# Attention tokens on 128 partitions in four and a half columns instead of 96 partitions in six

## The reference

```python
# 1. linear attention, per batch and head
q_s = softmax(q, axis=-1)              # over the 64 numbers of a token
k_s = softmax(k, axis=2)               # over the 576 tokens
attn = q_s @ (k_s.T @ v)               # x: [B, 576, 512]
# 2. token mixing, then channel mixing
h   = relu(x.T @ w_tok1) @ w_tok2      # 576 -> 256 -> 576 over tokens
u   = x + h.T
x1  = u + relu(u @ w_ch1) @ w_ch2      # 512 -> 1536 -> 512
# 3. experts: one of E = 8 per token
logits = x1 @ w_gate; local = sigmoid(x1 @ w_local)
# a token takes argmax(logits) if local < 0.5 (or it is the first), else the expert of the token before
out = softmax(logits)[e] * (relu(x1 @ w1[e]) @ w2[e])
```

## Time and profile before

| | us |
|---|---|
| median of three runs | 767.28 |
| lowest and highest | 767.22, 769.18 |
| profiled execution | 769.06 |
| its span, first to last instruction | 767.3 |

### The profile page before, as it was taken

The page is one execution under the profiler, slowest core; times in us unless marked ns, Lnnn a source line. Parts: engine busy times, 40 slices in busy tenths (PEclk is TensorE's granted clock), DMA queues, the critical chain, the costliest instruction groups (busy, mean ns, idle before and its releaser), DMA issues.

```text
span 767.3 us, 14091 instructions
## 1 busy us (share of the span) xinstructions
PE 748.6 (98%) x4836; PEld 682.4 (89%) x4837; DVE 310.0 (40%) x617; ACT 226.5 (30%) x401; POOL 141.7 (18%) x159
## 2 busy tenths in 40 slices
PE   6999999999999999999999999999999899999997
PEld 6979999999999999999999999977788688888885
DVE  6656251226241226251223643584624363222531
ACT  2753133113123104123103025221624362222531
POOL 6483030002020002020000015102312131212221
PEclk9999999999999999999999999999999999999999
DMA  9950305001405001401001240105723444101010
GB/s 206 372 92 14 81 14 111 1 2 32 94 1 124 1 1 33 93 1 32 1 1 37 81 153 31 52 28 196 266 80 122 159 164 137 49 27 49 18 35 12
DMA packets 67851, 57.62 MB, mean 75 GB/s; under 512 B 51356, under 2 KB 53116, under 8 KB 67808
## 3 DMA queue, kind: packets, MB, share of 16 engines
q1 hardware_dynamic: 64288, 47.57, 21.9%
q0 software_dynamic: 3520, 9.44, 3.7%
HBM read 48.79 MB, written 10.31 MB: 77 GB/s over the span
## 4 chain that ended last, share of the span: by engine, by line
PE 88%; DVE 5%; POOL 2%; ACT 1%; issue 1%; DMA 1%; DVEq 0%; ACTq 0%; SPq 0%; POOLq 0%
PE bank L583 38%; PE bank L729 14%; PE bank L704 14%; PE bank L525 5%; PE bank L554 4%; PE bank L716 2%; POOL qb L1611 2%; PE bank L497 2%; PE bank L548 2%; PE bank L593 1%; PE bank L604 1%; PE bank L652 1%; PE bank L513 1%; PE bank L535 1%; DVE qsum L1087 1%
## 5 line engine op out<-in xcount | busy, mean ns | idle before, releaser
L583 PE MATMUL bank<-u_h,wc_h 128*128 128x288 f32 x384 | 119.9, 312 | 0.0
L583 PE MATMUL bank<-hid_h,wc_h 128*128 128x288 f32 x384 | 116.9, 304 | 0.0
L583 PE MATMUL bank<-hid_l,wc_h 128*128 128x288 f32 x384 | 113.2, 295 | 0.0
L583 PE MATMUL bank<-u_l,wc_h 128*128 128x288 f32 x384 | 113.1, 294 | 0.0
L583 PE MATMUL bank<-hid_h,wc_l 128*128 128x288 f32 x384 | 113.0, 294 | 0.0
L583 PE MATMUL bank<-u_h,wc_l 128*128 128x288 f32 x384 | 113.0, 294 | 0.0
L704 PE MATMUL bank<-wslots,xgT_h 128*128 (+1 forms) x344 | 110.5, 402 | 0.4 <-issue 0.2
L729 PE MATMUL bank<-wslots,hT_h 128*128 (+1 forms) x336 | 105.1, 394 | 5.2 <-DVE hT_l L1504 5.2
L1331 DVE SCALAR_TENSOR_TENSOR hid_l<-bank,hid_h 128x288 fp32r<-128x288 f32 x96 | 43.4, 454 | 128.2 <-ACT hid_h L883 128.0
L729 PEld LDWEIGHTS bank<-wslots,hT_h 128*128 128x128 f32 x336 | 63.0, 189 | 19.9 <-issue 4.4
L883 ACT ACTIVATE hid_h<-bank 128x288 fp32r<-128x288 f32 x96 | 39.0, 408 | 124.7 <-PE bank L583 124.7
(11 more groups left out here) (247 smaller groups left out, 1080.4 us busy)
## 6 DMA issues: line engine op xcount, KB each, us to landing
w1raw<-in_moe_w_dram SPq DMA_DIRECT2D x20, 512.0 KB, 5.0
w2raw<-in_moe_w_dram SPq DMA_DIRECT2D x20, 512.0 KB, 3.7
wc_raw<-in_moe_w_ch_dram SPq DMA_DIRECT2D x8, 768.0 KB, 11.1
x_rows<-x1n SPq DMA_DIRECT2D x24, 192.0 KB, 2.1
kb<-in_k_dram SPq DMA_DIRECT2D x24, 144.0 KB, 3.4
qb<-in_q_dram SPq DMA_DIRECT2D x24, 144.0 KB, 3.3
vb_e<-in_v_dram SPq DMA_DIRECT2D x16, 144.0 KB, 3.9
vb_o<-in_v_dram SPq DMA_DIRECT2D x16, 144.0 KB, 3.7
```

The costliest lines, as they stand in the source:

```text
L583: last = pe.matmul(to, lhsT, rhs, start=(m == 0), stop=(m == len(mms) - 1))
```

## The change

Tokens stand on all 128 partitions. The first 512 tokens of a batch fill four columns (partition p holds tokens 4p to 4p+3), and the last 64 stand on partitions 0 to 63 of a fifth column. `TOP` = 4 is that column's number, `FULL` = 512, `REST` = 64. The parts of the softmaxes are now columns 0 to 1 and 2 to 4. Products over tokens use 128 rows for four columns and 64 for the fifth (`tokens_on`). In `qT` the tokens now stand as two halves of 256 + 32, in order of the token within each: the half with tokens 0 to 255 and 512 to 543, and the one with 256 to 511 and 544 to 575. ACT's copies out of PSUM do this ordering, and the rows of a half come out as two blocks of 128 and one of 32 in plain token order.

The core of the diff, with the rest left out:

```diff
-    PS = 96
-    NI = S // PS
-    HI = NI // 2
+    NI = -(-S // P)
+    TOP = NI - 1
+    FULL = TOP * P
+    REST = S - FULL
+    HB = 3
+    NB = 2 * HB
...
-        IHALF = (slice(0, HI), slice(HI, NI))
+        IHALF = (slice(0, 2), slice(2, NI))
+        BLOCKS = ((0, P), (P, P), (2 * P, REST // 2))
+        def tokens_on(i):
+            return P if i < TOP else REST
...
             def load_raw(dst, src, g, b, landed):
-                sp.dma_start(dst[:, g, :, :, :].rearrange("p h i d -> p h (i d)"),
-                             src[b, g * HG:(g + 1) * HG, :, :].rearrange("h (p i) d -> p h (i d)", p=PS)).then_inc(landed, 16)
+                heads = src[b, g * HG:(g + 1) * HG, :, :]
+                sp.dma_start(dst[:, g, :, 0:TOP, :].rearrange("p h i d -> p h (i d)"),
+                             heads[:, 0:FULL, :].rearrange("h (p i) d -> p h (i d)", p=P)).then_inc(landed, 16)
+                sp.dma_start(dst[0:REST, g, :, TOP, :], heads[:, FULL:S, :].rearrange("h p d -> p h d")).then_inc(landed, 16)
...
             def store_logits(b):
                 sp.wait_ge(lg_done, 2 * b + 3)
-                rows = lg_rows.rearrange("(b p i) r -> b p (i r)", b=B, i=NI)
-                rows = rows[bass.ds(b, 1), :, :].rearrange("a p n -> (a p) n")
-                sp.dma_start(rows, lgs[:, :, :].rearrange("p i r -> p (i r)")).then_inc(lg_stored, 16)
+                for half in range(2):
+                    at = b * S + block_row(half * HB)
+                    sp.dma_start(lg_rows[at:at + 2 * P, :].rearrange("(k p) r -> p k r", k=2), lgs[:, half, 0:2, :]).then_inc(lg_stored, 16)
+                    at, size = b * S + block_row(half * HB + 2), BLOCKS[2][1]
+                    sp.dma_start(lg_rows[at:at + size, :], lgs[0:size, half, 2, :]).then_inc(lg_stored, 16)
...
             def kv(n, g):
...
-                        last = pe.matmul(k_bank(n, g)[:, c * KV:(c + 1) * KV], keys(n)[:, i, c * P:(c + 1) * P], vb[g][:, 2 * c:2 * c + 2, i, :],
+                        last = pe.matmul(k_bank(n, g)[:, c * KV:(c + 1) * KV], keys(n)[0:tokens_on(i), i, c * P:(c + 1) * P], vb[g][0:tokens_on(i), 2 * c:2 * c + 2, i, :],
...
             def qT_out(n, g, tiles):
                 for j in tiles:
                     act.wait_ge(qT_ready, 4 * n + j + 1)
-                    act.activation(qT[:, g, j // 2, HS * (j % 2):HS * (j % 2) + HS], bank[4 + j % 2][:, 0:HS], ACT.Copy).then_inc(qT_done, 1)
+                    halves = qT[:, g, j // 2, :].rearrange("p (h s) -> p h s", h=2)
+                    in_order = halves[:, :, 0:2 * P].rearrange("p h (q i) -> p i h q", i=TOP)[:, 2 * (j % 2):2 * (j % 2) + 2, :, :]
+                    done = act.activation(in_order, bank[4 + j % 2][:, 0:2 * P].rearrange("p (i h q) -> p i h q", i=2, h=2), ACT.Copy)
+                    if j % 2:
+                        done = act.activation(halves[:, :, 2 * P:HS], bank[5][:, 2 * P:2 * P + REST].rearrange("p (h q) -> p h q", h=2), ACT.Copy)
+                    done.then_inc(qT_done, 1)
...
         def _(pool):
...
+            for i, raw in enumerate((qraw, kraw)):
+                pool.memset(raw[REST:P, :, :, TOP, :], 0.0).then_inc(padded, 1)
+                pool.wait_ge(padded, i + 1)
             make(pool.memset(ident[:, :], 0.0))
```

More of the change, by code:

```diff
@@ L278, in build @@
         LAST = B - 1
-        HEAD = HI
+        HEAD = HB
         CPIECE = KC // KD
@@ L413, in batch @@
                     load_kv(b + 2, 0)
-                for i in range(1, HI):
+                for i in range(1, HB):
                     store_rows(b, i)
@@ L418, in batch @@
                 store_logits(b)
-                for i in range(HI, NI):
+                for i in range(HB, NB):
                     store_rows(b, i)
@@ L511, in qT_tiles @@
                     c = j // 2
-                    for i in range(HI):
-                        last = pe.transpose(bank[4 + j % 2][:, i * PS:(i + 1) * PS],
-                                            queries(n)[:, HI * (j % 2) + i, c * P:(c + 1) * P], ident[0:PS, 0:PS])
+                    first = IHALF[j % 2].start
+                    for i in range(first, IHALF[j % 2].stop):
+                        on = tokens_on(i)
+                        last = pe.transpose(bank[4 + j % 2][:, (i - first) * P:(i - first) * P + on],
+                                            queries(n)[0:on, i, c * P:(c + 1) * P], ident[0:on, 0:on])
                     last.then_inc(qT_ready, 1)
@@ L590, in logits @@
                 pe.wait_ge(lg_done, 2 * b + half + 1)
-                for i in range(HI):
+                for i, (at, size) in enumerate(BLOCKS):
                     for c in range(KD):
-                        last = pe.matmul(bank[6][0:PS, i * R:(i + 1) * R], x1T[:, c, i * PS:(i + 1) * PS], wr[:, c, :],
+                        last = pe.matmul(bank[6][0:size, i * R:(i + 1) * R], x1T[:, c, at:at + size], wr[:, c, :],
                                          start=(c == 0), stop=(c == KD - 1))
@@ L597, in rows @@
             def rows(b, half, i):
-                part = slice(i * PS, (i + 1) * PS)
+                at, size = BLOCKS[i]
                 if i == 0:
                     logits(b, half)
-                pe.wait_ge(x1n_done, NI * b + HI * half + i + 1)
+                pe.wait_ge(x1n_done, NB * b + HB * half + i + 1)
                 for c in range(KD):
-                    last = pe.transpose(bank[7][0:PS, c * P:(c + 1) * P], x1T[:, c, part], ident[:, :])
+                    last = pe.transpose(bank[7][0:size, c * P:(c + 1) * P], x1T[:, c, at:at + size], ident[:, :])
                 last.then_inc(x1r_ready, 1)
@@ L616, in batch @@
                                 u_tile(b + 1, j)
-                    for i in range(HI):
+                    for i in range(HB):
                         if LX_AT[i] == idx:
@@ L857, in rows_out @@
             def rows_out(b, half, i):
-                at = HI * half + i
+                at, size = HB * half + i, BLOCKS[i][1]
                 if i == 0:
@@ L861, in rows_out @@
                     if half == 0:
-                        act.wait_ge(lg_stored, 16 * (b + 1))
-                    act.activation(lgs[:, HI * half:HI * half + HI, :].rearrange("p i r -> p (i r)"), bank[6][0:PS, 0:HI * R], ACT.Copy).then_inc(lg_done, 1)
-                act.wait_ge(x1r_ready, NI * b + at + 2)
-                act.wait_ge(x1_stored[at % 2], 16 * (HI * b + at // 2 + 1))
-                act.activation(x1n[:, at % 2, :], bank[7][0:PS, :], ACT.Copy).then_inc(x1n_done, 1)
+                        act.wait_ge(lg_stored, 64 * (b + 1))
+                    act.activation(lgs[:, half, 0:2, :].rearrange("p i r -> p (i r)"), bank[6][:, 0:2 * R], ACT.Copy)
+                    few = BLOCKS[2][1]
+                    act.activation(lgs[0:few, half, 2, :], bank[6][0:few, 2 * R:3 * R], ACT.Copy).then_inc(lg_done, 1)
+                act.wait_ge(x1r_ready, NB * b + at + 2)
+                act.wait_ge(x1_stored[at % 2], 16 * (HB * b + at // 2 + 1))
+                act.activation(x1n[0:size, at % 2, :], bank[7][0:size, :], ACT.Copy).then_inc(x1n_done, 1)
             def unit_hi(n, i, slot):
@@ L946, in _ @@
             for m in range(KT):
-                last = act.activation(wt2[:, m, :].rearrange("p (i s) -> p i s", i=NI),
-                                      wt2_raw[:, m, :].rearrange("p (s i) -> p i s", i=NI), ACT.Copy)
+                halves = wt2[:, m, :].rearrange("p (h s) -> p h s", h=2)
+                act.activation(halves[:, :, 0:2 * P], wt2_raw[:, m, 0:FULL].rearrange("p (h s) -> p h s", h=2), ACT.Copy)
+                last = act.activation(halves[:, :, 2 * P:HS], wt2_raw[:, m, FULL:S].rearrange("p (h s) -> p h s", h=2), ACT.Copy)
             last.then_inc(wt2_ready, 1)
@@ L1060, in ksub @@
                     dve.wait_ge(mb_ready, n + 1)
-                m = k_bank(n, g)[0:PS, 0:DG].rearrange("p (h d) -> p h d", h=HG).unsqueeze(1).broadcast_to([PS, HI, HG, DH])
+                if n == 0 and part == 1:
+                    dve.wait_ge(padded, 2)
+                layers = IHALF[part].stop - IHALF[part].start
+                m = k_bank(n, g)[:, 0:DG].rearrange("p (h d) -> p h d", h=HG).unsqueeze(1).broadcast_to([P, layers, HG, DH])
                 dve.tensor_tensor(by_head(keys(n))[:, IHALF[part], :, :], loaded(n, kraw, kb)[:, IHALF[part], :, :], m, ALU.subtract).then_inc(ksub_done, 1)
```

120 lines of the change are left out of this document (67 added, 53 removed).

## The result

The changed kernel takes 775.81 us (median of four, 775.52 to 778.12), the kernel before 768.23 us in the same session: ratio 1.010, 95% interval 1.0066 to 1.0134. It is slower by 7.6 us, where 7.9 us less were forecast. The profiled execution took 775.9 us, its span 774.2 (767.3 before). Times of one kernel move with the mean granted clock (the kernel before: 767.2 us at 0.997, 771.5 at 0.990, 774.5 at 0.986), so I compare stages by the traces as well.

The account below looks back on a forecast made before the run. PE was taken to bound the kernel from 54 to 490 us. Terms -7.86 + 0.8 + 0.9 - 0.5 - 1.2 = -7.9 us, from a median of 767.28 us, gave 759.4 us, range 755.8 to 764.5.

Parts of the forecast that it names:

- the first of the gain: Key and mixing products: five blocks for six save 1.31 us per head group, -7.86 us for six groups inside batches.
- Query turns: Turns of queries on PE: the same 1152 columns, about 0.50 us again, so 0.
- Router and row turns: Router products in blocks of 128, 128 and 32: +0.9 us, bounds -0.4 to +3.0; row turns 0.
- Key turn and spread: Turn of the key maximum and its spread widen from 96 to 128: +0.8 us over eight groups.
- ScalarE and loads: Strided copies of turned queries, 0.64 us each, covered in batches: 0; loads 0 there, at most +0.2 us per first load.
- POOL: POOL's scaling in batches: its first part gets a third shorter, so PE's 0.17 us wait goes, -0.5 us over three batches.
- The logits' four stores: End of batches: three more issues, about +1.1 us, taken up by DVE's later idle; 0, bound +1.
- The head: From 0 to 54 us: first key products 0.7 us later, then 1.9 us saved; -1.2 us, bounds -3.5 to +3.
- D: Rival: one half-clock stretch fewer in the head (1.7 us) and cheap pads (1.5 us), 756.2 us; chance 0.09.
- C: Rival: no saving, as ten products with 128 rows last as long as twelve of 96; 767.3 us, chance 0.06.
- A: Rival: in the head, first loads are paid by pieces, first key maximum 4.7 us late; 763.4 us, chance 0.12.
- B: Rival: ACT's strided copies at 2.1 us each stall PE in three batches, 15 us lost; 774.4 us, chance 0.05.

Follow-up runs that it names:

- the padded kernel: Changed kernel with the fifth column's key and mixing products and query turns padded to 128 rows, router blocks unchanged: 758.30 us, ratio 0.9859 to the kernel before.
- blocks_96: Changed kernel with only the router's products and row turns back in three blocks of 96 rows: 775.62 us, ratio 1.0080 to the kernel before.
- micro_more: Changed kernel with further series of 16 products of varied rows, columns, places and lengths behind the warming ones; 64 with 128 rows, 512 moving columns: 0.196 us a change.

## Why the prediction was wrong

- **The failed step** is the first of the gain: "A column block of tokens costs a product as many moving columns whether 96, 128 or 64 partitions hold data". For one product it holds (3.84 against 3.79 us for sixteen). Between products it does not: each 64-row product among 128-row ones changes the form twice, 0.39 us. The saving was sized exactly, -2.62 us a batch, as the padded kernel shows (-2.63), and eight 64-row products gave 3.07 back. The prediction had priced the product and not its neighbour; the warning it needed was that no row of the trace held two forms in turn.
- **Query turns**, counted 0, cost +1.10 us a batch for the same reason (2.92 for 1.82 without waits), padded +0.11 (1.93). The ledger's +0.52 hides this, as 0.58 us of waits go in the same row. (The prediction's "three with half of one" should be four and half of one; its 0.50 us is right for that.)
- **Router and row turns.** +0.24 forecast, +0.43 measured. The 32-column products have starts 31 to 32 ns apart (I took 50, bounds 27 to 82), but the surplus is the changes on entering and leaving.
- **Key turn and spread**: +0.2 a batch forecast, +0.05 measured; the spread stayed at 0.44 us in the chain, its lower bound.
- **ScalarE and loads** came as forecast, POOL better. PE's waits for POOL within batches are gone (all 1.6 us that are left lie in the head), which gives 0.58 us a batch: the 0.17 of idle time that the prediction read leaves out what hides behind the records' modelled ends. The strided copy took 658 ns, near the wt2 row's price (0.64), though that row's stride was on the read and this one is on the write. The first k landed at 8.39 us for 8.21. The Trainium skill, "SBUF — State Buffer", section "Door 1: The DMA port swizzle", by which a stride of four fp32 is free, is not borne out for ScalarE's writes: 381 ns contiguous, 658 with the stride. The logits' four stores delay the load back by 1.5 us (1.1 forecast), and PE never waits for them:
```profile
495.66 0.37 SPq L394 DMA_DIRECT2D lg_rows<-lgs  x1
...
499.17 0.34 SPq L467 DMA_DIRECT2D lg<-lg_rows  x1
```
- **The head** came out at +1.3 instead of -1.2, in two halves: PE is 0.65 us late, and DVE's last split takes 0.7 us longer. Its chain after, against the earlier trace rows:
```profile
1.40 0.53 POOL kraw L1625
...
4.01 7.50 PE bank L495 x96
11.51 0.24 PE bank L502 x2
...
14.25 2.48 POOL qb L1657 x2
...
17.45 0.64 ACT qT L855
...
19.98 3.78 PE bank L519 x20
...
25.37 4.91 PE bank L549 x20
30.27 3.01 PE bank L519 x20
...
47.48 0.46 DVE u_l L1143
47.94 2.80 DVE wc_l L1415
```
and of before:
```profile
30.18 2.68 PE bank L497 x24
...
46.83 0.46 DVE u_l L1101
```
Pads and scaling cost what was forecast, the warming 0.6 us less, and the key products start at 19.98 as before, not 0.7 later. From there the 1.9 us of saving is absent: 3.78 us for twenty records where twenty-four took 3.72, and 3.01 for 2.68 in the second group. The `u_l` ahead of the split starts 0.65 us late. The split `wc_l`, the same instruction in both kernels, then takes 2.80 us of the chain for 2.10, and PE's wait for `u_l` grows from 0.7 to 1.4 us. In the heads of the runs this instruction lasts between 1.8 and 3.4 us, each time with POOL's splits of other weights beside it; no run tests what made it longer here.
- **The sum and the rivals.** The last 1.5 us are in the experts, counted 0. A half-clock stretch was put at 1.7 us, but the two rows given for it, 3.72 and 2.68 us, make 1.0; D rests on it. C named the right outcome for its term (no saving) with the wrong cause: 128 rows are not slower. A and B did not happen. D's full clock did not come in the changed kernel (0.84 and 0.82 from 15 to 25 us). None spoke of neighbours with different forms, and the chance of 0.88 for faster was too high for a change that puts an operand shape into the kernel that no row had shown.

## What to carry to other kernels

When a blocking leaves a short last block, price the switch as well as the product: here two changes of form cost an fp32 product 0.39 us, where a key product itself takes 0.22 and a mixing product 0.43. Pad the operand with zeros to the neighbours' form (eight products a batch and three small memsets took 2.7 to 3.0 us off each batch here), or, where that can't be, set the short products side by side. Full blocks in a less full form (96 rows) among 128-row products are free.

## What the runs showed of the hardware

- The form follows the count coarsely: 72, 96 and 128 rows go together (106 to 107 ns from record to record for 72 with 128 in bf16 at half clock, 3.79 us a series for 96 with 128), 64 does not (6.69 us), nor 32; 96 and 128 stationary columns go together (3.75 us), while 64 and 32 do not (6.27 and 6.05).
- At full clock an fp32 product pays at both of its records, about 0.1 us each, a bf16 product at its one. The bf16 price is 0.11 us at half clock as well (128 with 32 rows: 215 to 220 ns for 107, where at full clock 157 to 163 stand for 56).
- Two 64-row tiles at partitions 0 and 64, into two banks, run side by side (2.06 us against 3.79 for sixteen fp32 products).
- A stride of 16 bytes on ScalarE's writes costs about 0.28 us per 256 elements.
- The head's low-clock stretch came and went with small shifts of work. From 20 to 25 us the granted clock was 0.82 in the changed kernel and 0.50 in blocks_96, which differ first at the router products, after 100 us, and 1.00 with padded turns. In micro_more it went from 1.00 (13 to 15 us) to 0.50 (from 17.6) while PE had no idle time. What sets it stays open.
